# Even pairs' scores split by parts of the sequence, gate logits in column tiles, the mask loaded first

## The reference

```python
# attention: a local query sees the keys within 32 positions and the 32 global keys
s_g = scale * q_g @ k_all.T;  out_g = sm(s_g) @ v_all
s_ll = where(|i - j| <= 32, scale * q_l @ k_l.T, -1e9);  s_lg = scale * q_l @ k_g.T
out_l = sm(concat([s_lg, s_ll])) @ concat([v_g, v_l])
# expert layer: logits = x @ w_gate (8 experts), local_gate = sigmoid(x @ w_local)
# a position with local_gate >= 0.5 keeps the expert of the position before it
out[b, s] = p[e] * (relu(x[b, s] @ w1[e]) @ w2[e])
# conv layer
h = relu(x @ w_in); out = (h * sigmoid(conv3(h))) @ w_out
```

## Time and profile before

| | us |
|---|---|
| median of 3 runs (lowest to highest) | 692.94 (689.23 to 694.88) |
| the profiled execution's own time | 693.83 |
| its span, first to last instruction | 692.0 |
| attention loop, first group's `scores` to the first transposes of routing | 13.15 to 147.88 |
| transposes and gate logits | 147.88 to 173.4 |
| serial routing steps | 173.4 to 197.2 |
| expert layer and conv layer | 197.2 to 692 |

### The profile page before, as it was taken

One profiled execution on the slowest core, in us unless ns is written; L12 is line 12 of the kernel. 1 busy time (PEld: TensorE's weight loads), 2 busy tenths in 40 slices (PEclk: granted clock), 3 DMA queues, 4 the chain that ended last, 5 costly groups with the idle time before them and its releaser, 6 DMA issues.

```text
span 692.0 us, 14269 instructions
## 1 busy us (share of the span) xinstructions
PE 650.1 (94%) x4737; PEld 518.5 (75%) x4737; DVE 505.8 (73%) x1001; ACT 355.6 (51%) x567; POOL 196.6 (28%) x160
## 2 busy tenths in 40 slices
PE   3888888899889999999999999998999999999997
PEld 3666666664667888888888888886788888888886
DVE  2665656553858899998989989884489777787772
ACT  2555656541037787877878777783333232321321
POOL 2000000034154555545555555541412020000000
PEclk9999999999889999999999999999999999999999
DMA  8764647238811117163614435400411021100102
GB/s 303 235 212 145 213 143 224 106 123 329 324 62 31 49 44 288 45 239 133 234 45 151 167 114 220 167 16 32 112 41 47 1 91 30 61 0 0 61 1 76
DMA packets 37946, 85.03 MB, mean 123 GB/s; under 512 B 7952, under 2 KB 8976, under 8 KB 37904
## 3 DMA queue, kind: packets, MB, share of 16 engines
q1 hardware_dynamic: 29776, 61.39, 25.8%
q0 software_dynamic: 4960, 17.30, 7.5%
q10 hardware_dynamic: 3168, 5.77, 2.2%
HBM read 69.25 MB, written 15.20 MB: 122 GB/s over the span
## 4 chain that ended last, share of the span: by engine, by line
PE 90%; DVE 5%; DMA 1%; issue 1%; ACT 1%; SPq 1%; POOL 0%; DVEq 0%; POOLq 0%; ACTq 0%
PE ps L858 21%; PE ps L859 21%; PE ps L860 21%; PE ps L699 3%; PE ps L889 3%; PE ps L695 3%; PE ps L669 3%; PE ps L636 2%; PE ps L769 2%; PE ps L672 1%; DVE l_p L1039 1%; PE ps L867 1%; PE ps L637 1%; PE ps L811 1%; PE ps L944 1%
## 5 line engine op out<-in xcount | busy, mean ns | idle before, releaser
L1446 ACT CAST w_h<-slots 128x1024 fp32r x88 | 92.0, 1048 | 46.5 <-issue 23.4
L1452 ACT CAST w_h<-slots 128x1024 fp32r x88 | 89.5, 1050 | 39.2 <-PE ps L860 23.4
L1244 DVE TENSOR_TENSOR w_l<-slots,w_h 128x1024 fp32r<-128x1024 f32 x66 | 88.1, 1384 | 9.9 <-ACT w_h L1446 7.2
L1251 DVE TENSOR_TENSOR w_l<-slots,w_h 128x1024 fp32r<-128x1024 f32 x66 | 77.9, 1233 | 15.7 <-ACT w_h L1452 15.7
L1527 ACT ACTIVATE h_buf<-ps 128x512 f32<-128x512 f32 x32 | 19.2, 601 | 123.8 <-PE ps L860 108.7
L529 POOL TENSOR_TENSOR w_l<-slots,w_h 128x1024 fp32r<-128x1024 f32 x22 | 54.3, 2469 | 72.6 <-ACT w_h L1446 72.6
L858 PE MATMUL ps<-w_h,b_hTh 128*128 128x512 f32 x176 | 71.5, 406 | 2.6 <-DVE b_hTl L1238 2.6
L858 PE MATMUL ps<-w_h,b_xTh 128*128 128x512 f32 x176 | 70.5, 401 | 0.9 <-DVE w_l L1244 0.6
L860 PE MATMUL ps<-w_h,b_hTl 128*128 128x512 f32 x176 | 69.5, 395 | 0.0
L859 PE MATMUL ps<-w_l,b_hTh 128*128 128x512 f32 x176 | 69.3, 394 | 0.0
L860 PE MATMUL ps<-w_h,b_xTl 128*128 128x512 f32 x176 | 68.8, 391 | 0.0
(11 more groups left out here) (230 smaller groups left out, 1394.8 us busy)
## 6 DMA issues: line engine op xcount, KB each, us to landing
slots<-w SPq DMA_DIRECT2D x16, 2048.0 KB, 12.3
l_va<-va SPq DMA_DIRECT2D x16, 520.0 KB, 4.1
l_k<-kw SPq DMA_DIRECT2D x16, 352.0 KB, 3.4
y_sorted<-b_y ACTq DMA_DIRECT2D x22, 256.0 KB, 2.9
l_q<-ql SPq DMA_DIRECT2D x16, 256.0 KB, 3.6
x_rows<-X POOLq DMA_DIRECT2D x4, 1024.0 KB, 5.4
out<-o_l SPq DMA_DIRECT2D x4, 1024.0 KB, 4.3
win<-w_in POOLq DMA_DIRECT2D x1, 2048.0 KB, 12.2
```

The lines of the kernel that those rows point to most:

```text
L1244: vec.tensor_tensor(w_l[:, u, :], unit_of(at, False, u), w_h[:, u, :].bitcast(F32), ALU.subtract).then_inc(w_lo_dve, 1)
L1251: vec.tensor_tensor(w_l[:, u, :], unit_of(at, True, u), w_h[:, u, :].bitcast(F32), ALU.subtract).then_inc(w_lo_dve, 1)
L1446: sca.copy(w_h[:, u, :], unit_of(at, False, u)).then_inc(w_hi, 1)
L1452: sca.copy(w_h[:, u, :], unit_of(at, True, u)).then_inc(w_hi, 1)
```

## The change

- **Scores by halves.** `scores(pair, half)` does tiles 0, 1 (half 0) or 2, 3 (half 1), of both heads; the bank is now `2*half + u`, so half 0 fills banks 0 and 1 and half 1 banks 2 and 3. `negated_max` and `exponentials` also go by half and head (same instructions in number). For an even pair after the first, half 1 comes first, a turn and a weigh earlier than before; it waits only for the pair before; half 0 comes where the whole stood, and waits for the global exponentials. An odd pair's halves wait each for the same half of the pair before. DVE's and ACT's orders follow.
- **Loads.** The mask's columns of `consts` are loaded by SP right behind pair 0's keys; pair 0's queries and the rest of `consts` by ACT. SP loads keys and queries one pair ahead of values and waits for no clearing. The block loads `l_vg` move to POOL's queue: behind the clearing for pairs 0 to 5, and for 6 to 15 each after `o_ready`, between the stores of the batches.
- **Logits.** `gate_w` is padded to 32 columns; chunk c of the four goes to partitions 32c to 32c+31 without accumulation, and `turn_logits` becomes a matmul with a 0/1 matrix (`C_SUM`) that turns and adds the four.

The diff, cut to its core:

```diff
@@ -424,20 +455,22 @@
         @block.sync
         def _(sp):
             load_keys(sp, 0)
-            sp.dma_start(consts[:], cst).then_inc(const_in, 16)
-            sp.wait_ge(vg_zero, 1)
-            load_values(sp, 0)
-            for pair in range(1, NRING):
-                load_keys(sp, pair)
-                sp.wait_ge(vg_zero, pair + 1)
-                load_values(sp, pair)
+            sp.dma_start(consts[:, C_MASK:NC_CONST], cst[:, C_MASK:NC_CONST]).then_inc(mask_in, 16)
+            for pair in range(NRING):
+                if pair >= 1:
+                    load_keys(sp, pair)
+                    load_queries(sp, pair)
+                if pair >= 1:
+                    load_values(sp, pair - 1)
                 if pair == 1:
                     sp.dma_start(g_q[:], qg).then_inc(gq_in, 16)
+            load_values(sp, NRING - 1)
             sp.dma_start(gate_w[:], wg).then_inc(gate_in, 16)
             sp.dma_start(conv_w[:], cw).then_inc(gate_in, 16)
             for pair in range(NRING, NPAIR):
                 sp.wait_ge(o_ready, sub_g((pair - NRING) // 2) + 1)
                 load_keys(sp, pair)
+                load_queries(sp, pair)
                 load_values(sp, pair)
             sp.wait_ge(o_ready, SUBS)
...
@@ -489,8 +525,11 @@
                 pool.dma_start(x_rows[SL * b:SL * b + SL, :].rearrange("(t p) d -> p t d", p=P),
                                X[:, NT * b:NT * b + NT, :]).then_inc(rows_stored, 16)
-            for b in range(B - 1):
-                store_batch(b)
+            for pair in range(NRING, NPAIR):
+                pool.wait_ge(o_ready, sub_g((pair - NRING) // 2) + 1)
+                load_blocks(pool, pair)
+                if pair % (H // 2) == 3:
+                    store_batch(pair // (H // 2) - 1)
             pool.dma_start(win[:], w_in.rearrange("(c p) f -> p c f", p=P)).then_inc(win_in, 16)
             store_batch(B - 1)
             pool.wait_ge(g_normed, NG)
...
@@ -618,25 +657,29 @@
-            def scores(pair):
-
-                i = pair % NRING
+            def scores(pair, half):
+
+                i, two = pair % NRING, range(2)
                 pe.wait_ge(qk_in[i], 32 * (pair // NRING + 1))
-                if pair >= 1:
-                    pe.wait_ge(max_ready, sub(pair - 1, 1) + 1)
-                    if pair % 2 == 0:
-                        pe.wait_ge(p_ready, sub_g(pair // 2 - 1) + 1)
-                for t in range(NT):
+                if pair % 2 == 1:
+                    pe.wait_ge(max_ready, maxed(pair - 1, half, 1))
+                elif pair and half == 1:
+                    pe.wait_ge(max_ready, maxed(pair - 1, 1, 1))
+                elif pair:
+                    pe.wait_ge(p_ready, sub_g(pair // 2 - 1) + 1)
+                for t in range(2 * half, 2 * half + 2):
                     at = t % 2 * TK
-                    q = [slice(P * t + HQ * h, P * t + HQ * h + HQ) for h in range(2)]
-                    rows = [slice(DH * u, DH * u + DH) for u in range(2)]
+                    q = [slice(P * t + HQ * h, P * t + HQ * h + HQ) for h in two]
+                    rows = [slice(DH * u, DH * u + DH) for u in two]
                     k = l_k[i][:, TK * t:TK * t + TK]
                     beside = l_k[i][:, TK * t + HQ:TK * t + TK + HQ + SG].rearrange("p (a k) -> p a k", a=2)[:, :, 0:HQ]
-                    for u, r in enumerate(rows):
-                        mm(ps[0:HQ, 2 * u + t // 2, at:at + TK], l_q[i][r, q[0]], k[r], start=True, stop=True)
-                        mm(ps[HQ:P, 2 * u + t // 2, at:at + WK], l_q[i][r, q[1]], beside[r], start=True, stop=True)
-                    for u, r in enumerate(rows):
-                        last = mm(ps[HQ:P, 2 * u + t // 2, at + WK:at + TK], l_q[i][r, q[1]], k[r, WK:TK],
+                    for u in two:
+                        r, bank = rows[u], 2 * half + u
+                        mm(ps[0:HQ, bank, at:at + TK], l_q[i][r, q[0]], k[r], start=True, stop=True)
+                        mm(ps[HQ:P, bank, at:at + WK], l_q[i][r, q[1]], beside[r], start=True, stop=True)
+                    for u in two:
+                        r = rows[u]
+                        last = mm(ps[HQ:P, 2 * half + u, at + WK:at + TK], l_q[i][r, q[1]], k[r, WK:TK],
                                   start=True, stop=True)
                 last.then_inc(s_ready, 1)
...
@@ -717,23 +761,28 @@
                                       start=False, stop=True)
                 last.then_inc(o_ready, 1)
-            scores(0)
+            for half in range(2):
+                scores(0, half)
             pe.wait_ge(const_in, 16)
             for g in range(NG):
-                for a in range(2):
-                    if a == 0:
-                        scores(2 * g + 1)
-                    else:
-                        g_scores(g)
-                    turn(2 * g + a, 0)
-                    if a == 1:
-                        weigh(2 * g, 1)
-                    elif g >= 1:
-                        g_weigh(g - 1)
-                    turn(2 * g + a, 1)
-                    weigh(2 * g + a, 0)
+                for half in range(2):
+                    scores(2 * g + 1, half)
+                turn(2 * g, 0)
+                if g >= 1:
+                    g_weigh(g - 1)
+                turn(2 * g, 1)
+                weigh(2 * g, 0)
+
+                g_scores(g)
+                turn(2 * g + 1, 0)
+                weigh(2 * g, 1)
                 if g + 1 < NG:
-                    scores(2 * g + 2)
+                    scores(2 * g + 2, 1)
+                turn(2 * g + 1, 1)
+                weigh(2 * g + 1, 0)
+
+                if g + 1 < NG:
+                    scores(2 * g + 2, 0)
                 g_turn(g)
                 weigh(2 * g + 1, 1)
             g_weigh(NG - 1)
@@ -766,15 +815,15 @@
                     pe.wait_ge(lt_copied, g - 1)
                 n = P * len(tiles)
                 for c in range(DC):
-                    last = mm(ps[0:E + 1, 6 + g % 2, 0:n], gate_w[:, c, :], r_xT[g % 2][:, c, 0:n],
-                              start=(c == 0), stop=(c == DC - 1))
+                    last = mm(ps[32 * c:32 * c + 32, 6 + g % 2, 0:n], gate_w[:, c, :], r_xT[g % 2][:, c, 0:n],
+                              start=True, stop=True)
                 last.then_inc(lt_ready, 1)
             def turn_logits(g):
                 pe.wait_ge(lt_copied, g + 1)
                 for tile in tiles_of[g]:
-                    last = nc.tensor.transpose(ps[:, 5, (E + 1) * tile:(E + 1) * (tile + 1)],
-                                               r_lT[:, P * tile:P * tile + P], consts[0:E + 1, C_ID:C_ID + E + 1])
+                    last = mm(ps[:, 5, (E + 1) * tile:(E + 1) * (tile + 1)], r_lT[:, P * tile:P * tile + P],
+                              consts[:, C_SUM:C_SUM + E + 1], start=True, stop=True)
                 return last
             turn_tiles(0)
...
@@ -1074,39 +1123,43 @@
                 dve.wait_ge(gden_ready, g + 1)
                 vec.reciprocal(g_inv[:, g:g + 1], g_den[:, g:g + 1]).then_inc(ginv_ready, 1)
+            dve.wait_ge(mask_in, 16)
+            for half in range(2):
+                for u in range(2):
+                    negated_max(0, half, u)
             dve.wait_ge(const_in, 16)
-            for u in range(2):
-                negated_max(0, u)
             vec.tensor_copy(identb[:], ident)
             vec.tensor_copy(laneb[:], consts[:, C_LANE:C_LANE + P])
             for g in range(NG):
-                for a in range(2):
-                    pair = 2 * g + a
-                    if a == 0:
-                        negated_max(pair + 1, 0)
-                    else:
-                        g_negated_max(g)
-                    copy_turned(sub(pair, 0))
-                    if a == 1:
-                        normalize(pair - 1, 1)
-                    elif g >= 1:
-                        g_inverse(g - 1)
-                    if a == 0:
-                        negated_max(pair + 1, 1)
-                    normalize(pair, 0)
+                for u in range(2):
+                    negated_max(2 * g + 1, 0, u)
+                copy_turned(sub(2 * g, 0))
+                if g >= 1:
+                    g_inverse(g - 1)
+                for u in range(2):
+                    negated_max(2 * g + 1, 1, u)
+                normalize(2 * g, 0)
+
+                g_negated_max(g)
+                copy_turned(sub(2 * g + 1, 0))
+                normalize(2 * g, 1)
                 if g + 1 < NG:
-                    negated_max(2 * g + 2, 0)
+                    for u in range(2):
+                        negated_max(2 * g + 2, 1, u)
+                normalize(2 * g + 1, 0)
+
+                if g + 1 < NG:
+                    for u in range(2):
+                        negated_max(2 * g + 2, 0, u)
                 copy_turned(sub_g(g))
                 normalize(2 * g + 1, 1)
-                if g + 1 < NG:
-                    negated_max(2 * g + 2, 1)
```

(100 more changed lines are left out.)

6 lines of the change are left out of this document (3 added, 3 removed).

## The result

| | before | changed |
|---|---|---|
| median beside each other, us | 693.31 (689.23 to 694.88, 4 runs) | 666.80 (664.95 to 667.74, 4 runs) |
| ratio, 95% interval | | 0.9623 [0.9577, 0.9669] |
| the profiled execution's span | 692.0 | 665.6 |

A forecast was written before the change was run, and what follows sets the result against it. TensorE, busy 94% of the span, was taken as the bound. Loop 15.3, with the start 20.3, plus routing 7.1 made 27.4 us; taken from the profiled 693.83 or the median 692.94, that gave 666 us, range 658 to 677.

The forecast's parts named there:

- The sum: Whole kernel: 20.3 us from loop and start plus 7.1 from routing, a gain of 27.4 us.
- The wait and where it goes: Attention loop: seven 2.0 us waits of TensorE for DVE's `negated_max` go, 14.0 us; groups of 14.8 us.
- ACT's path into turn(2g+1,0): Attention loop: this turn waits for exponentials behind `g_normalize` and copies, 0.2 us late per group, bounds 0 and 0.6.
- the drain of two bursts: Even pair's scores in the loop: two separate bursts each drain the quarters, 0.2 us per group, bounds 0 and 0.5.
- The clock in the loop: Attention loop: with no gap over 0.3 us left, none of three clock falls remains, gaining 4.3 us.
- The start: Before pair 1's scores: earlier loads let them begin at 8.1 us, gain 5.0, bounds 2.5 and 5.6.
- Logits: Routing's gate logits: column tiles take 1.0 us for 3.53 per batch, gain 10.1; with the end together 10.6.
- column tiles run one after the other: Routing's logits: a rule read from the skill page, gain nothing; rival of half or no overlap, 671 to 673, chance 0.10.
- The collision with the third load: First gather after routing: issued inside the third weight load, it lands 3.5 us later, bounds 0 and 4.2.
- a fall in the first block: First block of rows: a possible clock fall there as earlier work shifts, given no size of its own.
- Block loads on POOL: 64 block loads moved to POOL's queue at 0.91 us an issue, cost 0; rival of a slower queue, chance 0.03.
- The open term: Routing at clock 0.50 from about 183 to 193: 3 us less possible, or a fall in the first block.

The follow-up runs named there:

- ACT's order: The changed kernel with ACT's `g_normalize` taken behind the first head's second pair of exponentials; 665.80 us, beside the changed kernel's 667.17.

## Why the prediction was right, point by point

**The sum: luck in part.** The total is closer than its parts. The logits gave 2.2 us less than forecast and the loop 0.9 less; against that stand 1.2 us in the serial steps, which no term of the sum had, and 1.0 of the gather.

**The wait and where it goes: right.** The 2.0 us were DVE's `negated_max` of the second head behind a copy and `normalize`; the old order with all else new has them again, 14.0 in seven groups. The group came out at 14.6 to 14.7 for 14.8. Of the two additions, ACT's path into turn(2g+1,0) is real: the 0.2 us wait stands in the profile and goes with ACT's order (14.44). The other, 0.2 for the drain of two bursts, was too much: 16.39 - 2.0 is 14.39, and 14.44 is what is left when ACT is out of the way, so 0.05.

**The clock in the loop: right.** In ten profiled executions without the gaps no group had a fall; with them two in the rebuilt old order, for three in the kernel before; with fillers in them, none, in the one execution profiled.

**The start: right for the transfers, incomplete after them.** Pair 1's scores at 8.37 for 8.1. What the sum left out is that the first group itself varies by 2.8 us with the level of the clock, and the profiled execution of the result had the bad case. That, not the steady groups, is why the loop gave 14.4 and not 15.3: the other seven groups alone gave 14.7, and in the second profiled execution of the changed kernel the loop gave 17.1.

**Logits: the matmuls right, the turn back missed.** 1.00 for 1.0. The sum priced the new `turn_logits` at nothing, without a sentence; a transpose had become a plain fp32 matmul, 0.99 for 0.34 three times and 1.23 for 0.58 at the end, 2.6 us in all. 10.6 should have been 8. The row that would have told it was there: transposes of 128 columns (L669) take one record each, matmuls of as many columns (L672) two.
The Trainium skill's sentence on row groups ("TensorE: Matmul & The Clock Gate", Part 3, Packing small matmuls) is on weight loads: they overlap matmuls in flight only when the row group differs. The prediction concluded from it that column tiles run one after the other; that went beyond the sentence, as the table of the same part gives a measured speedup for three column tiles. Nor does the sentence hold here: four matmuls of 512 columns in tiles that share all rows take 1.00 us, against 3.53 one behind the other, and the weight loads of all four fall inside the first matmul's time (135.82 to 136.44). The measurement decides: column tiles overlap here.

**The collision with the third load: right.** Predicted in place and cause; 6.1 us for a predicted 7.0. Holding that load back gives 3.5, and the lower level in the first block goes as well, a second cost of the same wait that the prediction had only as "a fall in the first block".

**Block loads on POOL: right.** 0.54 us an issue for the 0.91 taken, and no wait of `weigh` for them.

**The open term.** Routing's time at half clock moved, from one stretch of 10.2 us to two of 6.9 and 3.4, so its amount stayed the same. The serial steps gained 1.2 us; some of them (L834 and L841, 1.87 and 1.85 us in the kernel before) now lie outside the half level and take 1.05 and 1.01, but that this makes the 1.2 is not shown.

## What to carry to other kernels

A handover that frees only half of a double buffer can be cut along another axis, so that both sides work on what the third party leaves free; walk the other engines' order for the new halves as well, since here ACT's next item became the limit by 0.2 us. After a stage is shortened, look for loads that run on a clock of their own and now overlap the first transfer of the next stage. When an instruction changes its form, a transpose to a matmul even with nine columns, it needs a price of its own.

## What the runs showed of the hardware

- With 9 columns moving, an fp32 transpose takes one record, 0.085 us in a row of four; a plain fp32 matmul two, 0.245 us, with 9 rows or 128.
- Four 512-column fp32 matmuls in four column tiles take 1.00 us for 3.53.
- Gaps of 2.0 us in a loop of 16.4 us brought the granted clock to half for 3.4 us behind three of seven gaps in one kernel and two of seven in another; with matmuls in the gaps, or with no gaps, it never fell in the loop, in eleven profiled executions.
- The trace's granted clock starts with a rise, at 9.0 to 24.1 us in executions without filler matmuls at the start and at 5.6 in the two with them; before it, where the stretches read 1.00, records are up to 1.7 times as long.
- The same program's first group took 13.7, 13.8 or 16.4 us from pair 1's scores to the first global turn.
